# Four mixes of a tile behind one product, tanh gates, and attention woven into the first chunk of a fused attention and gated convolution kernel

## The reference

```
scores = q k^T / sqrt(D) - slope_h * |i - j|   where 0 <= i - j < 128, else -1e9
x  = softmax(scores) v                          # batch 4, 8 heads, 576 rows, head 64

h  = relu(x @ w_in)                             # 512 -> 1024
g1 = h * sigmoid(conv3(h))                      # taps at -1, 0, +1 rows
x2 = g1 @ w_out                                 # 1024 -> 512

g2 = sigmoid(conv5(x2)) * (x2 @ w_val)          # causal, 5 taps, 512 -> 512
y  = g2 @ w_out2                                # 512 -> 512
```

## Time and profile before

| | |
|---|---|
| median of 3 runs | 470.3 us (468.93 to 470.31) |
| profiled execution | 470.26 us, its span 468.5 us |
| busy in the span | PE 442.6, DVE 320.3, ACT 297.1, POOL 82.3 us |
| mean granted clock of TensorE | 0.978 of full speed |
| table loads on ACT | 16, of 1.28 us each |
| mean ns of one, on ACT | Relu L459 397, centre tap L468 502, exp L420 432 and its read of the sum 188, sigmoid L474 437 |
| mean ns of one, on DVE | guard L577 178, L565 325, inverse L585 160, normalise L597 338, side tap L650 513, gate product L658 450, `low_of_panel` L620 834 |

### The profile page before, as it was taken

How to read it: one execution, slowest core, us unless ns; L and a number is a source line. 1 busy time by engine, 2 the same in 40 slices (tenths; PEclk the granted TensorE clock), 3 DMA queues, 4 the chain that set the end, 5 groups by cost and what they waited for, 6 DMA issues and landing times.

```text
span 468.5 us, 9674 instructions
## 1 busy us (share of the span) xinstructions
PE 442.6 (94%) x3376; PEld 410.3 (88%) x3376; DVE 320.3 (68%) x1128; ACT 297.1 (63%) x916; POOL 82.3 (18%) x116
## 2 busy tenths in 40 slices
PE   4888579997999999999999999999999999999997
PEld 3668558996889998999889998999889998899997
DVE  7795895976685767757776667847778475847760
ACT  3686953386667975398566976488666876377132
POOL 3310990044000220013000230014000140004000
PEclk9999857999999999999999999999999999999999
DMA  8865102001211012011210112121211100010002
GB/s 212 222 199 214 45 15 78 1 1 45 69 47 38 25 46 68 27 49 46 70 45 27 37 25 67 37 62 42 57 45 44 36 2 1 2 50 2 1 14 88
DMA packets 38928, 25.81 MB, mean 55 GB/s; under 512 B 22752, under 2 KB 35040, under 8 KB 38880
## 3 DMA queue, kind: packets, MB, share of 16 engines
q1 hardware_dynamic: 38880, 25.20, 18.7%
HBM read 20.47 MB, written 4.72 MB: 54 GB/s over the span
## 4 chain that ended last, share of the span: by engine, by line
PE 81%; DVE 7%; ACT 5%; issue 2%; DMA 1%; POOL 1%; SPq 1%; DVEq 0%; ACTq 0%
PE bank L827 20%; PE bank L828 20%; PE bank L829 20%; PE bank L808 8%; PE bank L778 8%; PE bank L788 6%; DVE probs L597 1%; DMA k_all<-k_t 1%; DVE probs L565 1%; ACT conv L468 1%; DVE gate L706 1%; DVE conv L650 1%; DVE w_lo L620 1%; ACT conv L474 1%; ACT bank L459 1%
## 5 line engine op out<-in xcount | busy, mean ns | idle before, releaser
L827 PE MATMUL bank<-g_hi,w_hi 128*128 128x288 f32 x384 | 121.2, 316 | 0.0
L827 PE MATMUL bank<-x_hi,w_hi 128*128 128x290 f32 (+1 forms) x384 | 114.3, 298 | 3.7 <-DVE x_lo L640 1.4
L828 PE MATMUL bank<-g_lo,w_hi 128*128 128x288 f32 x384 | 114.0, 297 | 0.0
L828 PE MATMUL bank<-x_lo,w_hi 128*128 128x290 f32 (+1 forms) x384 | 113.6, 296 | 0.0
L829 PE MATMUL bank<-g_hi,w_lo 128*128 128x288 f32 x384 | 113.6, 296 | 0.0
L829 PE MATMUL bank<-x_hi,w_lo 128*128 128x290 f32 (+1 forms) x384 | 113.3, 295 | 0.0
L389 POOL TENSOR_TENSOR g_lo<-conv,g_hi 128x288 fp32r<-128x288 f32 x64 | 51.9, 812 | 330.7 <-ACT g_hi L482 330.7
L650 DVE SCALAR_TENSOR_TENSOR conv<-bank,taps,conv 128x288 f32<-128x288 f32 (+1 forms) x128 | 65.5, 513 | 53.6 <-ACT conv L468 53.4
L420 ACT ACTIVATE probs<-probs,neg_max 128x192 f32<-128x192 f32 (+2 forms) x144 | 62.0, 432 | 28.9 <-DVE neg_max L565 28.4
L827 PEld LDWEIGHTS bank<-x_hi,w_hi 128*128 128x128 f32 x384 | 72.4, 188 | 4.6 <-DVE conv L658 1.8
L827 PEld LDWEIGHTS bank<-g_hi,w_hi 128*128 128x128 f32 x384 | 72.8, 190 | 0.8 <-issue 0.5
(11 more groups left out here) (49 smaller groups left out, 542.9 us busy)
## 6 DMA issues: line engine op xcount, KB each, us to landing
w_raw<-panels SPq DMA_DIRECT2D x12, 512.0 KB, 5.9
y_t<-y_sb SPq DMA_DIRECT2D x32, 144.0 KB, 1.7
q_tile<-q_t SPq DMA_DIRECT2D x32, 128.0 KB, 3.0
k_all<-k_t SPq DMA_DIRECT2D x16, 256.0 KB, 3.7
v_tile<-v_tiles SPq DMA_DIRECT2D x16, 256.0 KB, 2.7
q_tile<-q_t SPq DMA_DIRECT2D x8, 64.0 KB, 2.4
k_all<-k_t SPq DMA_DIRECT2D x4, 128.0 KB, 2.6
v_tile<-v_tiles SPq DMA_DIRECT2D x4, 128.0 KB, 3.0
```

The costliest lines, as they stand in the source:

```text
L827: pe.matmul(out, w_hi[:, p, col:col + P], hi(k), start=start, stop=False)
L828: pe.matmul(out, w_hi[:, p, col:col + P], lo(k), start=False, stop=False)
```

## The change

- `T_RING = 4` buffers of `probs_t` instead of 2. PE's `close` does nothing after the first three steps of a tile and all four mixes after the fourth.
- The six steps 12 to 17 go into beats 2 to 7 of chunk 0 (`WOVEN`), between its up products; only 18 and 19 run alone, before beat 9. The up products of chunk 0 use banks 0 to 3 in turn and wait for `g1_done` of the block four before; its down products take banks 0 and 1 in turn, first halves first. In the woven beats ACT does the copies, then Relu and the centre tap, then the exps.
- Both sigmoids become tanh: sigmoid(x) = (1 + tanh(x/2)) / 2. Relu is scaled by 0.5, DVE's gate product becomes (tanh + 1) * bank, and the last copy is scaled by 0.5.
- `low_of_panel` for halves 8 to 15 moves into DVE's beats 0 to 7 of chunk 0; `round_panel` of panels 4 to 7 into POOL's beats 0 to 3; the splits of panels 10 and 11 into beats 10 and 14 of chunk 1.

```diff
+T_RING = 4
+WOVEN = 6
-        probs_t = [place(f"probs_t{r}", [P, 4 * P]) for r in range(2)]
+        probs_t = [place(f"probs_t{r}", [P, 4 * P]) for r in range(T_RING)]
+        def up_bank(c, m):
+            return UP_BANK[m] if c > 0 else m % KM
+        def down_of(c, j):
+            n = j - DOWN0
+            if c == 0 and n < KM:
+                return n % 2, n // 2
+            return n // 2, n % 2
         def last_of_run(step):
-            return step % STEPS in (FIRST - 1, STEPS - 1)
+            return step % STEPS in (FIRST - 1, STEPS - 1) and step != FIRST - 1
         def step_at(c, j):
+            if c == 0 and KW - WOVEN <= j < KW:
+                return FIRST + j - KW + WOVEN
...
-                    if c == 0 and j == VAL0 + 2:
-                        run(slot, close, range(FIRST, STEPS))
+                    if c == 0 and j == VAL0 + 1:
+                        run(slot, close, range(FIRST + WOVEN, STEPS))
...
# POOL
             def beat(c, j, step):
+                if c == 0 and j < P_VAL - P_OUT:
+                    round_panel(P_OUT + j)
                 if c < CHUNKS and 2 <= j < KW + 2:
                     g1_low(c, j - 2)
-                if c == 0 and j < KW and j % 2 == 1:
-                    round_panel(P_OUT + j // 2)
                 if c == 0 and j in (DOWN0, DOWN0 + 4):
                     split_panel(P_VAL + (j - DOWN0) // 4)
-                if c == 1 and j in (0, 4):
-                    split_panel(P_OUT2 + j // 4)
+                if c == 1 and j in (KW + 2, KW + 6):
+                    split_panel(P_OUT2 + (j - KW) // 4)
...
# ACT
-                reach(act, mixed, step - 1)
-                to = probs_t[step % 2]
+                reach(act, mixed, step - T_RING + 1)
+                to = probs_t[step % T_RING]
...
-                act.activation(bank[:, 0:READ], bank[:, 0:READ], ACT.Relu).then_inc(hidden_done, 1)
+                act.activation(bank[:, 0:READ], bank[:, 0:READ], ACT.Relu, scale=0.5).then_inc(hidden_done, 1)
...
-                               ACT.Sigmoid).then_inc(gate1_done, 1)
+                act.activation(conv[n % DEPTH][:, :], conv[n % DEPTH][:, :], ACT.Tanh).then_inc(gate1_done, 1)
...
-                act.activation(gate2[:, m, :], gate2[:, m, :], ACT.Sigmoid).then_inc(gate2_done, 1)
+                act.activation(gate2[:, m, :], gate2[:, m, :], ACT.Tanh, scale=0.5).then_inc(gate2_done, 1)
...
             def beat(c, j, step):
-                if step is not None:
+                if step is not None and j < KW:
+                    turned_rows(step)
+                elif step is not None:
                     slot(step)
                 if c < CHUNKS and j < KW:
                     hidden_rows(c, j)
                 if c < CHUNKS and j < KW:
                     center_rows(c, j)
+                if step is not None and j < KW:
+                    exps(step + LOOK - 1)
...
# DVE
-                if 0 <= step - STEPS + 2 * P_VAL < 2 * P_VAL:
-                    low_of_panel(step - STEPS + 2 * P_VAL)
+                if FIRST - 2 * P_OUT <= step < FIRST:
+                    low_of_panel(step - FIRST + 2 * P_OUT)
...
-                dve.tensor_tensor(conv[n % DEPTH][:, :], banks[UP_BANK[m]][:, at:at + HALF],
-                                  conv[n % DEPTH][:, :], ALU.mult).then_inc(g1_done, 1)
+                dve.scalar_tensor_tensor(out=conv[n % DEPTH][:, :], in0=conv[n % DEPTH][:, :], scalar=1.0,
+                                         in1=banks[up_bank(c, m)][:, at:at + HALF], op0=ALU.add,
+                                         op1=ALU.mult).then_inc(g1_done, 1)
...
                 if j <= KW:
                     up_beat(c, j)
+                if c == 0 and j < 2 * (P_VAL - P_OUT):
+                    low_of_panel(2 * P_OUT + j)
...
# PE
+            def close(step):
+                if step % PAIRS == PAIRS - 1:
+                    for n in range(step - PAIRS + 1, step + 1):
+                        mix(n)
...
-                if bank >= KM:
+                if c == 0:
+                    reach(pe, g1_done, m - KM + 1)
+                elif bank >= KM:
                     attention_left(c - 1, bank)
...
-                        pe.wait_ge(g1_done, UP_BANK.index(m) + 1)
+                        pe.wait_ge(g1_done, KM + m + 1)
...
-                    down(c, (j - DOWN0) // 2, (j - DOWN0) % 2)
+                    down(c, *down_of(c, j))
...
-            walk(slot, mix, beat)
+            walk(slot, close, beat)
```

More of the change, by code:

```diff
@@ L425, in slot, with turned_rows @@
             def slot(step):
+                turned_rows(step)
+                if step + LOOK - 1 < ALL_STEPS:
+                    exps(step + LOOK - 1)
+            def turned_rows(step):
                 _, t, _ = where(step)
                 act.wait_ge(turned, step + 1)
-                reach(act, mixed, step - 1)
-                to = probs_t[step % 2]
+                reach(act, mixed, step - T_RING + 1)
+                to = probs_t[step % T_RING]
                 if 0 < t < FULL:
@@ L441, in slot @@
                 act.copy(to[0:SUB, 2 * P:3 * P], t_ps[0:SUB, P:2 * P]).then_inc(copied, 1)
-                if step + LOOK - 1 < ALL_STEPS:
-                    exps(step + LOOK - 1)
             def close(step):
@@ L456, in hidden_rows @@
             def hidden_rows(c, m):
-                bank = banks[UP_BANK[m]]
+                bank = banks[up_bank(c, m)]
                 act.wait_ge(up_done, KW * c + m + 1)
-                act.activation(bank[:, 0:READ], bank[:, 0:READ], ACT.Relu).then_inc(hidden_done, 1)
+                act.activation(bank[:, 0:READ], bank[:, 0:READ], ACT.Relu, scale=0.5).then_inc(hidden_done, 1)
             def center_rows(c, m):
@@ L467, in center_rows @@
                 reach(act, g1_lo_done, n - DEPTH + 1)
-                act.activation(conv[n % DEPTH][:, :], banks[UP_BANK[m]][:, at:at + HALF], ACT.Copy,
+                act.activation(conv[n % DEPTH][:, :], banks[up_bank(c, m)][:, at:at + HALF], ACT.Copy,
                                scale=taps1[:, 1, m:m + 1]).then_inc(center_done, 1)
@@ L473, in gate_rows @@
                 act.wait_ge(conv_done, n + 1)
-                act.activation(conv[n % DEPTH][:, :], conv[n % DEPTH][:, :],
-                               ACT.Sigmoid).then_inc(gate1_done, 1)
+                act.activation(conv[n % DEPTH][:, :], conv[n % DEPTH][:, :], ACT.Tanh).then_inc(gate1_done, 1)
             def g1_high(c, m):
@@ L505, in out_rows @@
                 reach(act, y_stored[n % Y_RING], 16 * (n // Y_RING))
-                act.copy(y_sb[n % Y_RING][:, :], banks[out_bank(c, m)][:, 0:HALF]).then_inc(y_kept, 1)
+                act.activation(y_sb[n % Y_RING][:, :], banks[out_bank(c, m)][:, 0:HALF], ACT.Copy,
+                               scale=0.5).then_inc(y_kept, 1)
             def beat(c, j, step):
-                if step is not None:
+                if step is not None and j < KW:
+                    turned_rows(step)
+                elif step is not None:
                     slot(step)
@@ L520, in beat @@
                     g2_high(c - 1, j - VAL0)
-                if c < CHUNKS and DOWN0 <= j < OUT0 and j % 2 == 1:
-                    x2_high(c, (j - DOWN0) // 2)
+                if c < CHUNKS and DOWN0 <= j < OUT0 and down_of(c, j)[1] == 1:
+                    x2_high(c, down_of(c, j)[0])
                 if out_of(c, j):
@@ L650, in side_tap @@
                 dve.scalar_tensor_tensor(
-                    out=out, in0=banks[UP_BANK[m]][:, at + skip_first:at + HALF - skip_last],
+                    out=out, in0=banks[up_bank(c, m)][:, at + skip_first:at + HALF - skip_last],
                     scalar=taps1[:, tap, m:m + 1], in1=out, op0=ALU.mult, op1=ALU.add).then_inc(
@@ L674, in val_rows @@
                 dve.wait_ge(gate2_done, n + 1)
-                dve.tensor_tensor(gate2[:, m, :], banks[val_bank(c, m)][:, 0:HALF], gate2[:, m, :],
-                                  ALU.mult).then_inc(g2_done, 1)
+                dve.scalar_tensor_tensor(out=gate2[:, m, :], in0=gate2[:, m, :], scalar=1.0,
+                                         in1=banks[val_bank(c, m)][:, 0:HALF], op0=ALU.add,
+                                         op1=ALU.mult).then_inc(g2_done, 1)
             def g2_low(c, m):
@@ L801, in mix @@
                 subs = len(halves_of(t))
-                turned_probs = probs_t[step % 2][:, :].rearrange("p (j a h i) -> p a j h i", a=2, j=2, h=2)
+                turned_probs = probs_t[step % T_RING][:, :].rearrange("p (j a h i) -> p a j h i", a=2, j=2, h=2)
                 for j in range(2 - blocks, 2):
@@ L854, in up @@
                 b, half = c // 2, c % 2
-                at, bank = first_row(half), UP_BANK[m]
+                at, bank = first_row(half), up_bank(c, m)
                 if m == 0:
```

## The result

The change makes the kernel slower, by less than one per cent: 471.71 us (median of 14 runs, 470.0 to 473.23) against 468.23 (14 runs, 466.44 to 470.8), ratio 1.0066 [1.0044, 1.0089]. On another chip it was 1.005 [1.0021, 1.008]. The forecast was 465.5 and faster.

What follows compares the result with a forecast made beforehand. PE sets the pace but idles in chunks 0 and 1; gapless after 121 us, it has only 0.2 us slack on VectorE's normalise. 470.26 + 0.5 + 1.5 - 4.2 - 2.6 = 465.5 us, range 456 to 472.5.

Steps and rivals of the forecast that it cites:

- part 2: Head, steps 0 to 11: grouped mixes, waiting copies and the panel cast together cost +1.5 us, bounds 0 and +2.5.
- part 4: Chunk 1: matches chunk 3's time once panel splits move, less the cost of splits beside attention; -2.6 us, bounds -3.8 and -1.
- The sum's base, 470.26: Whole kernel: time in us of the profiled execution before the change, to which all predicted terms were added.
- Part 1: Tiles outside chunk 1: grouping saves PE time but PE then waits for VectorE's normalise; +0.5 us, bounds -10.5 to +3.3.
- the wait of the copy of step 4: Head: ScalarE's wait for the first mix at step 4 takes back 0.9 us of the 1.4 saved.
- the copy of step 8 and the cast: Head: the copy waits for a mix, +0.9 us; panel 5's cast falls into VectorE's busy time, +0.6.
- The last term: End of the head: the last x_hi waits for four mixes instead of two, +0.5 us.
- Part 3: Chunk 0: six woven beats of 4.2 us, then steps 18 and 19 about 5.6; -4.2 us, bounds -9.0 and -0.6.
- within this figure: Chunk 0: the sigmoid's table load of 1.28 us disappears, counted inside the woven beat's 4.2 us.
- The -3.4: Chunk 1: its stretch up to the turn of step 24 falls from 31.10 us to chunk 3's 27.66.
- The one on the slower side: Woven beats of chunk 0: POOL and VectorE block each other, 5.35 us per beat, +6.9, total 472.4 us; chance 0.14.
- The one with the excursions all won: Steps 20 to 79: all 42 saved switches between products and mixes win 0.25 us each, 10.5, total 454.5; chance 0.12.

Runs made afterwards that it cites:

- e4: Kernel before the change, with four mixes together everywhere and four turned-probabilities buffers with their extra memsets added: 477.37 us, ratio 1.0207.
- e15: e10 with the sigmoid function called in place of tanh in both gates: 471.94 us, ratio 1.0091.
- e9: Changed kernel with, from step 20 on, VectorE's x_lo of a tile moved behind the next step's normalises: 460.34 us, ratio 0.9815.
- e6: Changed kernel with the splits of the last two panels back in beats 0 and 4 of chunk 1: 472.37 us, ratio 1.012.
- e11: Changed kernel with six turned-probabilities buffers in place of four and all their memsets on GpSimd: 467.96 us, ratio 0.998.
- e5: Changed kernel with the eight memsets of the turned-probabilities buffers on GpSimd in place of VectorE: 471.4 us, ratio 1.009.
- e16: e13 with the memsets of the turned-probabilities buffers on GpSimd besides: 452.99 us, ratio 0.9684.
- e14: Changed kernel with a mix behind each step and no step woven, tanh gates and moved panel work kept: 461.9 us, ratio 0.9871.
- e18: Kernel before the change with the change's panel work alone moved; sigmoid, one mix behind each step, nothing woven: 465.92 us, ratio 0.9961.
- e1: Changed kernel with the grouping undone, each mix behind its own step everywhere: 464.02 us, ratio 0.9923.
- e13: e10 with the splits of the last two panels moved from chunk 1 to beats 20 and 22 of chunk 0: 452.97 us, ratio 0.968.
- e2: Changed kernel with four mixes together only from step 20 on, each mix behind its own step before that: 465.71 us, ratio 0.9966.
- e8: Changed kernel with a mix behind each step and four second-convolution taps cut to 16 columns each: 461.61 us, ratio 0.9883.
- e10: e2 with, from step 20 on, VectorE's x_lo of a tile moved behind the next step's normalises: 454.41 us, ratio 0.9692.

## Why the prediction was wrong

The head (part 2) and chunk 1 (part 4) turned a forecast gain of 4.8 us into a loss of 1.6. By its own steps, against the profiled executions:

- **The sum's base, 470.26.** 2.0 us above the median of before's 14 runs. Three runs hid how far its executions differ; the change would have had to win 2 us to look like no change.
- **Part 1, the steady tiles: right, mechanism and size.** Predicted +0.5, measured -0.68 up to step 79 and +1.53 behind it, +0.85. By tile: heavy ones +0.42 and +0.40 (+0.43 predicted), first of an even chunk -0.91 (-0.75), second +0.76 (+0.35), first of chunk 3 -0.51 (-0.4), last +0.92 (+0.5). In the tiles from 121.83 us on PE waits 17 times for the normalise, 8.6 us in all, where 20 to 30 times were said. Two things are not in it. The other table loads were put at nothing, and with the mixes together they are worth some 3 us (e4, and e15's 3.6). And what I missed most stood in my own rows: VectorE's 2.99 us of idle time ahead of x_lo is not a fact of the work but of a place in a queue, and moving that one instruction (e9) turns the part's +0.85 into -10.5.
- **Part 2, the head: the step that failed.** Predicted +1.5, measured +4.75. Up to the turn of step 5 -0.5 was said and +0.54 came (19.84 to 20.38): the four extra memsets on VectorE, which put the first turn 1.08 us later, were left out of the sum, and the wait of the copy of step 4 took 1.1 where 0.9 stood. From there to the turn of step 11 +1.5 was said (the copy of step 8 and the cast) and +1.74 came, so these two terms were near. The last term failed: "+0.5" for an x_hi that waits for four mixes, and +2.47 came. With the clock up it is 0.87 (4.51 us from the turn of step 11 to the first up product in e6, 4.50 in e11, 3.64 before); the other 1.6 is the granted clock, 0.57 of full speed, which the prediction weighed for chunk 0 alone and put at nothing here. Six buffers (e11) take 3.7 of the 4.75 away, the fall of the clock with it. That the memsets cost nothing in the end is shown for the first turns by e5 and for a head with a mix behind each step by e16.
- **Part 3, chunk 0: near in size, wrong in cause.** -4.2 predicted, -3.5 measured, beats of 4.27, 4.22, 3.66, 4.32, 3.08 and 3.61 us where 4.2 was said. Two errors cancel in it: the six beats took 23.16 us and not 25.2, and steps 18 and 19 with their group 8.26 (68.89 to 77.15) and not 5.6. The clock did as said, 1.00 in the woven beats and 0.59 behind them, though two pauses (1.51 and 1.74 us) were longer than the 1.5 said. But without any weaving chunk 0 is shorter still (e14). The way from 38.26 to 34.74 is -1.3 for the moved panel work (e18), -4.7 for the tanh, the earlier place of the run and what else e14 has (not told apart), +0.8 for the weaving (e1) and +1.6 for the grouping. I had the tanh "within this figure" and the grouping in chunk 0 not at all. All of it starts from the long execution of before, so the -1.3 and the -3.5 may be smaller against a short one. A step whose total comes out right is not thereby shown.
- **Part 4, chunk 1: mis-sized.** -2.6 predicted, -0.8 measured. The price of the splits beside the steps was right (+1.2; e13 gets back 1.19). The -3.4 presumed that nothing else differs from chunk 3. Two things do: the first value product waits 0.9 us for g1 (L685 in the waits above), and the turn of step 24 stands behind a group, +0.4 (e1 to e2), where -0.4 was put: -3.4 + 1.2 + 0.9 + 0.4 = -0.9. The 0.9 is absent in e8, with less second convolution, and in e18, with the old order of down products (first up product to step 20: 16.35 us, in e14 17.21). So VectorE's convolution of chunk 0 ends late; that the new order of down products makes it so was not tried alone.
- **Rivals.** The one on the slower side, GpSimd and VectorE blocking each other in the woven beats, did not happen: no beat reached 5.0. The slower result came by no rival that I had, but by the head. The one with the excursions all won (-10.5, 454.5) is what the part from step 24 on gives once x_lo is out of the way: -10.5 in e9. That e10 as a whole takes 454.41 is luck, since its head, chunk 0 and chunk 1 are not those of that sum.

The error of +6.3 us in the profiled time is 3.2 head, 1.8 chunk 1, 0.7 chunk 0, 0.3 down products, 0.35 steady tiles and end.

## What to carry to other kernels

Work taken from the bounding engine is won only if nothing else it waits for was timed by that work. Where an engine is found idle ahead of an instruction that waits, with ready work queued behind it, move that instruction first and batch afterwards: alone the batching lost 6.7 us; with x_lo moved, the kernel with groups from step 20 on (e10) is about 10 us faster than the one without (e1), 0.9692 against 0.9923. Test a gain's cause by taking the credited part out, as with the weaving, before building on it.

## What the runs showed of the hardware

- Heads with groups and four buffers, whose longest pauses of PE are 2.0 to 2.3 us, had stretches with the granted clock near the 1.2 GHz level in five of six profiled executions, at places that differ, and in the changed kernel this cost 0.6 us on one group of 32 mixes and 1.6 up to the turn of step 12. Pauses of 1.51 and 1.74 us in its woven beats were followed by none.
- A table load of 1.28 us cost nothing where PE set the pace (e1 against before, steps 24 to 71), and 0.9 us of a light tile where it waited for VectorE (e4).
- Four mixes together take 1.97 us and one alone 0.66; with the pause into and out of them, a step without its mix is 2.63 us against 3.31.
- GpSimd's splits beside VectorE's normalise stretched a pair from 0.44 to 1.12 us; moved away, 1.19 us of PE's time came back. The Trainium skill (SBUF — State Buffer, Who interferes with whom) calls their shared port pair an exclusive lock; the stretch of 0.68 us, about one of GpSimd's subtracts of 0.7, agrees. Beside the up products of chunk 1 (e6) the splits cost 1.26 us more than beside the steps.
